# Low-weight products of the first layer on 49 rows each, in two halves of the array

## The chip, the cores and the metric

The kernel runs on one core of a Trainium2 chip. The metric is the device time of one execution, in microseconds (us); the kernel before takes 1061.57 us, the median of 3 runs (1059.65 to 1062.9). TensorE (PE) multiplies: it loads a stationary operand (the weights; the profile lists these loads as an engine of its own, PEld) and streams a moving operand past it. ScalarE (ACT) and VectorE (DVE) read its results from PSUM, in 8 banks, and write to SBUF.

## The reference

Two batches of 12480 tokens with 128 channels go through an attention with 49 agents, and its output goes through a layer with 2048 hidden features:

```python
a2k = sm(agents, k)          # softmax(scale * agents @ k.T), 49 x 12480
agent_v = a2k @ v            # 49 x 128
q2a = sm(q, agents)          # 12480 x 49
x = q2a @ agent_v
h = x @ w_in                 # 128 -> 2048
g = np.maximum(h, 0.0) + alpha * np.minimum(h, 0.0)
out = g @ w_out              # 2048 -> 128
```

## The kernel before

A first stage reads k and v, and forms `agent_v` of each batch. Since `h = q2a @ (agent_v @ w_in)`, the product M of `agent_v` and `w_in` (49 x 2048) is made once for each batch, so that the first layer has a contraction over 49 agents alone. To keep precision with float16 operands, M is split into a high and a low part, `M_a` and `M_b`, and so are the probabilities P. SBUF partitions 0 to 48 of `PT` hold the high part of P turned (agents by tokens), partitions 64 to 112 its low part (`LO` = 64, `A` = 49, `R` = 113). `M_a` holds the high part of M on both groups of partitions, `M_b` the low part on partitions 0 to 48, and zeros on the others, from a memset at the start. One product of 113 rows with `M_a` thus adds high x high and high x low, and one with `M_b` low x high.

The second stage, which takes most of the time, works through 52 chunks of 480 tokens. The features are 16 tiles of 128, in 8 pairs. For a pair PE issues, in the order in which the code is written: a wait for `lo_ready`, `first_layer` (L434: for the even and then the odd tile a product with `M_a` and one with `M_b`, each 480 columns long, into the banks 2g and 2g + 1), and `second_layer` of the pair two earlier (L442: six products of 128 rows by 480 columns: `w_hi`, `w_lo` with `r_hi`, and `w_hi` with `r_lo`, two of each). The increment of `h_ready` sits on the last product of `first_layer`. ACT then makes `r_hi` of both banks in one instruction (L614), and DVE `r_lo` (L825), whose increment of `lo_ready` lets PE write these banks again, two pairs later.

Once in a chunk, PE also issues the scores of the next chunk (L420, float32), the `linear` pair (L453), and four transposes of the split probabilities (L430, `stack`), which ACT copies from PSUM into `PT` (`query_out`, L604). That copy raises `q_ready`, for which PE waits ahead of the first layer of the next chunk and ahead of the scores. Every engine runs its instructions in the order written; loops (Fori) hold a body of two chunks.

A few products of the preparation have few rows and fall between those of the first chunk: L393 (`turn_values`, 49 rows), L399 (`values_max_row`, 49 rows, one column of weights), L404 (`values_max_everywhere`, one row) and L387 (`denominators`, 120 rows, 49 columns of weights).

Of the kernel before, what the change touches and what calls it, by code (L numbers as in the profile page):

```python
# [27 lines left out]
F16 = mybir.dt.float16  # L28
ALU = mybir.AluOpType
ACT = mybir.ActivationFunctionType  # L30
AX = mybir.AxisListType

B, N, C, A, F = 2, 12480, 128, 49, 2048
# [3 lines left out]
CHUNK = 4 * T  # L37
# [7 lines left out]
LO = 64  # L45
R = LO + A
# [6 lines left out]
def build(nc, kT, vP, qT, agT, w_in, w_inT, w_out, alpha_row, alpha_col, out):  # L53
    ctx = ExitStack()
    with ctx:
        def sb(name, shape, dt=F32):
            return ctx.enter_context(nc.sbuf_tensor(name, shape, dt))

        def sem(name):
            return ctx.enter_context(nc.semaphore(name))  # L60
# [44 lines left out]
        M_a = sb("M_a", [128, B, F], F16)  # L105
        M_b = sb("M_b", [128, B, F], F16)
# [13 lines left out]
        q_p = sb("q_p", [T, 4, A])  # L120
        stack = sb("stack", [T, 4, R], F16)
        PT = sb("PT", [128, 2, CHUNK], F16)
        r_hi = sb("r_hi", [128, RING, 2, CHUNK], F16)
        r_lo = sb("r_lo", [128, RING, 2, CHUNK], F16)
        y_lin = sb("y_lin", [C, 2, CHUNK])
# [5 lines left out]
        ps = ctx.enter_context(nc.psum_tensor("ps", [128, 8, 512], F32))  # L131
        OUT, LIN, SMALL = 4, 6, 7
# [25 lines left out]
        m_raw, m_high, m_low, l_raw, l_high, l_low = (  # L158
            sem(x) for x in ("m_raw", "m_high", "m_low", "l_raw", "l_high", "l_low"))

        q_scored, q_maxed, q_shifted, q_exped, q_summed, q_dened, q_reced, q_normed, q_hi, q_lo, q_turned, q_ready = (
            sem(x) for x in ("q_scored", "q_maxed", "q_shifted", "q_exped", "q_summed", "q_dened", "q_reced",
                             "q_normed", "q_hi", "q_lo", "q_turned", "q_ready"))
# [152 lines left out]
        def _(pe):  # L316
# [117 lines left out]
            def first_layer(g_even, p, half, b):  # L434
                for u in range(2):
                    f = 128 * (2 * p + u)
                    for w, last in ((M_a, False), (M_b, True)):
                        mm = pe.matmul(ps[:, 2 * g_even + u, 0:CHUNK], w[0:R, b, f:f + 128], PT[0:R, half, :],  # L438
                                       start=not last, stop=last)
                mm.then_inc(h_ready, 1)  # L440

            def second_layer(p, half):  # L442
# [8 lines left out]
            def linear(half, b):  # L451
                for w, last in ((L_a, False), (L_b, True)):
                    mm = pe.matmul(ps[:, LIN, 0:CHUNK], w[0:R, b, :], PT[0:R, half, :], start=not last, stop=last)  # L453
                mm.then_inc(lin_ready, 1)
# [28 lines left out]
            pe.wait_ge(m_low, 1)  # L483
            pe.wait_ge(l_low, 1)
            first_layer(0, 0, 0, 0)
            turn_values(1)
            first_layer(1, 1, 0, 0)

            pe.wait_ge(w_ready, 1)
# [60 lines left out]
        def _(act):  # L550
# [52 lines left out]

            def query_out(n, half):  # L604
                act.wait_ge(q_turned, n + 1)
                act.activation(PT[0:R, half, :], ps[0:R, SMALL, :].bitcast(F16)[:, 0:CHUNK], ACT.Copy).then_inc(q_ready, 1)

            def relu_hi(g, s, first):
                act.wait_ge(h_ready, g + 1)
# [50 lines left out]
        def _(dve):  # L660
# [93 lines left out]
            def values_max_top(b):  # L754
                dve.wait_ge(b_vrow, b + 1)
                then(dve.tensor_reduce(v_top[:, :], ps[0:1, AV_SMALL[b], 128:128 + A], AX.X, ALU.max))
                dve.tensor_scalar(v_top[:, :], v_top[:, :], TINY, None, ALU.max).then_inc(b_vtop, 1)
# [16 lines left out]
            def mixed_low(b, at, view, count):  # L774
                dve.wait_ge(m_high, count)
                n = view.shape[1]
                dve.tensor_tensor(M_b[0:A, b, at:at + n], view, M_a[0:A, b, at:at + n], ALU.subtract).then_inc(m_low, 1)

            def linear_low(b, bank):
                dve.wait_ge(l_high, b + 1)  # L780
                dve.tensor_tensor(L_b[0:A, b, :], ps[0:A, bank, 0:C], L_a[0:A, b, :], ALU.subtract).then_inc(l_low, 1)
# [5 lines left out]

            def mixed_low_first():
                linear_low(0, LIN)
                mixed_low(0, 0, ps[0:A, 0:4, :].rearrange("p f n -> p (f n)"), 1)  # L790

            def over_agents(x):
                return x.rearrange("p (t o) -> p t o", o=1).to_broadcast([T, 4, A])
# [3 lines left out]
            def query_shift(n):  # L797

                dve.wait_ge(q_scored, n + 1)
                dve.tensor_reduce(q_top[:, :], scores, AX.X, ALU.max).then_inc(q_maxed, 1)  # L800
                dve.wait_ge(q_maxed, n + 1)
                dve.tensor_tensor(q_e[:, :, :], scores, over_agents(q_top[:, :]), ALU.subtract).then_inc(q_shifted, 1)

            def query_sum(n):
                dve.wait_ge(q_exped, n + 1)
                dve.tensor_reduce(q_sum[:, :], q_e[:, :, :], AX.X, ALU.add).then_inc(q_summed, 1)
                dve.wait_ge(q_summed, n + 1)
                dve.tensor_scalar(q_den[:, :], q_sum[:, :], EPS, 1.0 / P_SCALE, ALU.add, ALU.mult).then_inc(q_dened, 1)
                dve.wait_ge(q_dened, n + 1)
                dve.reciprocal(q_rec[:, :], q_den[:, :]).then_inc(q_reced, 1)  # L810

            def query_norm(n):

                dve.wait_ge(q_reced, n + 1)
                dve.tensor_tensor(q_p[:, :, :], q_e[:, :, :], over_agents(q_rec[:, :]), ALU.mult).then_inc(q_normed, 1)

            def query_lo(n):
                dve.wait_ge(q_hi, n + 1)
                dve.tensor_tensor(stack[:, :, LO:R], q_p[:, :, :], stack[:, :, 0:A], ALU.subtract).then_inc(q_lo, 1)

            def relu_lo(g, s):

                dve.wait_ge(hi_ready, g + 1)
                e = s % 2
                dve.scalar_tensor_tensor(out=r_lo[:, s % RING, :, :], in0=ps[:, 2 * e:2 * e + 2, 0:CHUNK], scalar=0.0,  # L825
                                         in1=r_hi[:, s % RING, :, :], op0=ALU.max, op1=ALU.subtract).then_inc(lo_ready, 1)

            def finish(n, half, uses, unscale):

                dve.wait_ge(pair_done, PAIRS * n + PAIRS)  # L830
                dve.wait_ge(lin_saved, n + 1)
                if not (isinstance(uses, int) and uses == 0):

                    dve.wait_ge(stored[half], 16 * uses)
                dve.scalar_tensor_tensor(out=y[:, half, :], in0=ps[:, OUT + half, 0:CHUNK], scalar=unscale,
                                         in1=y_lin[:, half, :], op0=ALU.mult, op1=ALU.add).then_inc(y_ready, 1)
# [42 lines left out]
            def body(i, b, first, last):  # L879
                for half in range(2):  # L880
                    n = 2 * i + half
                    ahead = not (last and half == 1)
                    for p in range(PAIRS):
                        s = PAIRS * half + p
                        if p == 0 and ahead:
                            query_shift(n + 1)
                        if p == 1 and ahead:
                            query_sum(n + 1)
                            query_norm(n + 1)
                        if p == 2 and ahead:  # L890
                            query_lo(n + 1)
                        if ahead or p < PAIRS - 2:
                            relu_lo(2 * PAIRS * i + (s + 2), s + 2)
                        if isinstance(n, int) and n == 0:
                            if p == 1:
                                values_max_top(1)
                            if p == 2:
                                values_scaled(1)

                        if isinstance(n, int) and n == 0 and p == 4:  # L900
                            mixed_low(1, 3 * 512, ps[0:A, OUT + 1, :], 2)
                        if isinstance(n, int) and n < 3 and p == 5:
                            mixed_low(1, n * 512, ps[0:A, LIN, :], 3 + n)
                            if n == 0:
                                linear_low(1, SMALL)
                        if p == 3 and not (first and half == 0):

                            if half == 0:
                                finish(n - 1, 1, i - 1, prev_unscale[:, :])
                            else:  # L910
                                finish(n - 1, 0, i, out_unscale[:, b, :])
                        if p == 6 and half == 0 and not first:

                            dve.wait_ge(y_ready, n)
                            dve.tensor_copy(prev_unscale[:, :], out_unscale[:, b, :])
# [28 lines left out]
```

## Time and profile before

| | |
|---|---|
| median of 3 runs | 1061.57 us (1059.65 to 1062.9) |
| span of the profiled execution | 1057.5 us |
| PE busy, products | 1034.4 us (98%), 5800 instructions |
| PEld busy, weight loads | 579.0 us (55%) |
| DVE busy | 701.7 us (66%) |
| ACT busy | 518.5 us (49%) |
| one chunk of 480 tokens (602.77 to 620.39 us) | 17.62 us |

The profiled execution lists its span alone, 1057.5 us, from the first instruction of the program to the last; the median of the runs is 4.1 us above it, for what lies around the span. The shapes in a row read: `49*128` are the rows and columns of weights on the array, `49x113` the moving operand. The profile models the ends of products, and they overlap their successors; the distance from one start to the next tells what a product costs. Rows of the timeline merge equal neighbours (x2).

### The profile page before, as it was taken

The page shows a single profiled execution, that of the slowest core. Times are in us where ns is not written, and L with a number is a line of the kernel's source. Part 1 is how long each engine was busy: PE and PEld are TensorE (multiplying, and loading weights), DVE is VectorE, ACT ScalarE, POOL GpSimd, SP SyncE. Part 2 cuts the span into 40 slices and gives each one's busy share as a digit, 9 for nine tenths or more (in the row PEclk, how much of TensorE's full clock was granted, in tenths as well). Part 3 has the DMA queues.
Part 4 walks back from the last instruction along what each step waited for, and adds up shares of the span by engine and source line. Part 5 has one row for each costly group of instructions (what it writes and reads, how often), then busy time and mean ns, then how long its engine had stood idle before and what let it go on. Part 6 is the DMA issues. An engine that isn't in the chain of part 4 may idle for free.

```text
span 1057.5 us, 16185 instructions
## 1 busy us (share of the span) xinstructions
PE 1034.4 (98%) x5800; PEld 579.0 (55%) x5800; DVE 701.7 (66%) x991; ACT 518.5 (49%) x686; POOL 34.8 (3%) x27
## 2 busy tenths in 40 slices
PE   8978999999999999999999999999999999999998
PEld 8867855555555555555555555555555555555554
DVE  3686766666666666666666666666666666666665
ACT  2212355555555555555555555555555555555554
POOL 5070000000000000000000000000000000000000
PEclk9988999999999999999999999999999999999999
DMA  8877600101010101010101010101010101010100
GB/s 295 298 203 192 172 1 20 38 20 37 19 37 19 37 19 37 19 37 19 37 19 38 19 38 19 37 19 37 19 37 19 37 19 37 19 37 19 37 19 29
DMA packets 23116, 55.68 MB, mean 53 GB/s; under 512 B 2822, under 2 KB 16134, under 8 KB 22582
## 3 DMA queue, kind: packets, MB, share of 16 engines
q1 hardware_dynamic: 22806, 55.32, 17.0%
q8 instruction: 15, 0.25, 0.1%
q10 hardware_dynamic: 288, 0.06, 0.0%
q14 instruction: 7, 0.06, 0.0%
HBM read 42.59 MB, written 12.78 MB: 52 GB/s over the span
## 4 chain that ended last, share of the span: by engine, by line
PE 94%; DMA 3%; DVE 2%; ACT 0%; issue 0%; SPq 0%; DVEq 0%; ACTq 0%
PE ps L446 48%; PE ps L438 32%; PE ps L420 4%; PE ps L330 3%; PE ps L354 3%; PE ps L453 2%; DMA v_s<-vP 2%; PE ps L430 1%; DMA k_s<-kT 1%; PE ps L408 1%; DVE k_diag L689 1%; DMA agents<-agT 0%; DVE w_diag L729 0%; DVE S L699 0%; DVE r_lo L825 0%
## 5 line engine op out<-in xcount | busy, mean ns | idle before, releaser
L825 DVE SCALAR_TENSOR_TENSOR r_lo<-ps,r_hi 128x960 f16<-128x960 f32 x416 | 481.6, 1158 | 296.5 <-ACT r_hi L614 293.7
L614 ACT ACTIVATE r_hi<-ps 128x960 f16<-128x960 f32 x416 | 403.9, 971 | 431.5 <-PE ps L438 431.5
L438 PE MATMUL ps<-PT,M_a 113*128 113x480 f16 x832 | 304.3, 366 | 0.2 <-DVE r_lo L825 0.2
L438 PE MATMUL ps<-PT,M_b 113*128 113x480 f16 x832 | 303.0, 364 | 0.0
L446 PE MATMUL ps<-r_hi,w_hi 128*128 128x480 f16 x832 | 237.0, 365 | 0.0
L446 PE MATMUL ps<-r_lo,w_hi 128*128 128x480 f16 x832 | 236.5, 366 | 0.0
L446 PE MATMUL ps<-r_hi,w_lo 128*128 128x480 f16 x832 | 235.8, 365 | 0.0
L446 PEld LDWEIGHTS ps<-r_hi,w_hi 128*128 128x128 f16 x832 | 81.5, 98 | 87.5 <-DVE r_lo L825 0.3
L446 PEld LDWEIGHTS ps<-r_lo,w_hi 128*128 128x128 f16 x832 | 81.1, 97 | 87.4
L446 PEld LDWEIGHTS ps<-r_hi,w_lo 128*128 128x128 f16 x832 | 79.7, 96 | 89.0
L438 PEld LDWEIGHTS ps<-PT,M_a 113*128 113x128 f16 x832 | 83.5, 100 | 78.0 <-issue 0.5
L438 PEld LDWEIGHTS ps<-PT,M_b 113*128 113x128 f16 x832 | 81.1, 97 | 76.9 <-issue 0.7
L354 PE MATMUL ps<-v_s,e_s 120*49 120x128 f32 x416 | 52.6, 287 | 5.5 <-DMA v_s<-vP 3.3
L330 PE MATMUL ps<-agents,k_s 128*120 128x128 f32 x416 | 49.8, 284 | 7.1 <-DMA agents<-agT 4.6
L420 PEld LDWEIGHTS ps<-agents,q_s 128*120 128x120 f32 x416 | 51.7, 184 | 6.5 <-issue 0.2
L354 PEld LDWEIGHTS ps<-v_s,e_s 120*49 120x49 f32 x416 | 48.2, 131 | 9.0 <-DMA v_s<-vP 4.4
L330 PEld LDWEIGHTS ps<-agents,k_s 128*120 128x120 f32 x416 | 49.0, 193 | 7.5 <-DMA agents<-agT 4.6
L420 PE MATMUL ps<-agents,q_s 128*120 128x49 f32 x416 | 49.0, 261 | 0.0
L680 DVE TENSOR_REDUCE k_top<-S 120x49 f32<-120x392 f32 (+1 forms) x26 | 21.6, 833 | 30.3 <-ACT S L559 30.3
L572 ACT ACTIVATE e_s<-S 120x392 f32<-120x392 f32 (+1 forms) x26 | 13.6, 529 | 55.1 <-DVE S L699 51.1
L654 ACT ACTIVATE y_lin<-ps,lin_unscale 128x480 f32<-128x480 f32 x52 | 34.0, 654 | 0.0
L559 ACT ACTIVATE S<-ps 120x392 f32<-120x392 f32 (+1 forms) x26 | 12.9, 495 | 37.7 <-PE ps L330 37.7
(105 smaller groups left out, 452.5 us busy)
## 6 DMA issues: line engine op xcount, KB each, us to landing
k_s<-kT SPq DMA_DIRECT2D x26, 480.0 KB, 4.5
v_s<-vP SPq DMA_DIRECT2D x26, 480.0 KB, 5.6
q_s<-qT SPq DMA_DIRECT2D x52, 240.0 KB, 2.6
out<-y SPq DMA_DIRECT2D x52, 240.0 KB, 2.0
w_relu<-w_out SPq DMA_DIRECT2D x1, 1024.0 KB, 8.6
w_in_s<-w_in SPq DMA_DIRECT2D x1, 1024.0 KB, 7.5
w_inT_s<-w_inT SPq DMA_DIRECT2D x1, 1024.0 KB, 9.2
sigma<-alpha_row SPq DMA_DIRECT2D x1, 1024.0 KB, 8.3
```

What stands on the lines that cost most here:

```text
L330: mm = pe.matmul(ps[0:T, bank, t % 4 * 128:(t % 4 + 1) * 128], k_s[:, slot, t * T:(t + 1) * T], agents[:, :], start=True, stop=True)
L354: mm = pe.matmul(ps[0:A, AV[b], 0:C], e_s[:, slot, t * A:(t + 1) * A], v_s[:, slot, t * C:(t + 1) * C], start=(slot == RING and t == 0), s ...
L420: mm = pe.matmul(ps[0:T, SMALL, t * A:(t + 1) * A], q_s[:, half, t * T:(t + 1) * T], agents[:, b * A:(b + 1) * A], start=True, stop=True)
L438: mm = pe.matmul(ps[:, 2 * g_even + u, 0:CHUNK], w[0:R, b, f:f + 128], PT[0:R, half, :], start=not last, stop=last)
L446: mm = pe.matmul(ps[:, OUT + half, 0:CHUNK], w[:, 2 * p + u, :], r[:, s, u, :], start=(p == 0 and u == 0 and w is w_hi and r is r_hi), sto ...
L453: mm = pe.matmul(ps[:, LIN, 0:CHUNK], w[0:R, b, :], PT[0:R, half, :], start=not last, stop=last)
L559: act.activation(S[:, b, m, :].rearrange("p (t a) -> p t a", a=A), raw, ACT.Copy, scale=SCALE).then_inc(k_saved, 1)
L572: act.activation(e_s[:, slot, :], S[:, b, m, :], ACT.Exp).then_inc(k_exped, 1)
L614: act.activation(r_hi[:, s % RING, :, :], ps[:, 2 * e:2 * e + 2, 0:CHUNK], ACT.Relu).then_inc(hi_ready, 1)
L654: act.activation(y_lin[:, half, :], ps[:, LIN, 0:CHUNK], ACT.Copy, scale=lin_unscale[:, b, :]).then_inc(lin_saved, 1)
L680: dve.tensor_reduce(k_top[:, b, m, :], by_agent(S[:, b, m, :]), AX.X, ALU.max).then_inc(k_maxed, 1)
L825: dve.scalar_tensor_tensor(out=r_lo[:, s % RING, :, :], in0=ps[:, 2 * e:2 * e + 2, 0:CHUNK], scalar=0.0, in1=r_hi[:, s % RING, :, :], op0= ...
```

## The change

Three things change. In `first_layer` the two products with `M_a` come first, then the one with `M_b` of the even tile, on partitions 0 to 48, and then the one with `M_b` of the odd tile, on partitions 64 to 112. The odd one takes its moving operand from a new tile `PU`, whose partitions 64 to 112 hold a copy of the high part of P; ACT makes it in `query_out` by a second copy, which now carries the increment of `q_ready`. And the low part of M is made on all 113 partitions, by the same DVE instructions.

```diff
         PT = sb("PT", [128, 2, CHUNK], F16)
+        PU = sb("PU", [128, 2, CHUNK], F16)
...
             def first_layer(g_even, p, half, b):
                 for u in range(2):
                     f = 128 * (2 * p + u)
-                    for w, last in ((M_a, False), (M_b, True)):
-                        mm = pe.matmul(ps[:, 2 * g_even + u, 0:CHUNK], w[0:R, b, f:f + 128], PT[0:R, half, :],
-                                       start=not last, stop=last)
+                    pe.matmul(ps[:, 2 * g_even + u, 0:CHUNK], M_a[0:R, b, f:f + 128], PT[0:R, half, :],
+                              start=True, stop=False)
+                f = 256 * p
+                pe.matmul(ps[:, 2 * g_even, 0:CHUNK], M_b[0:A, b, f:f + 128], PT[0:A, half, :],
+                          start=False, stop=True)
+                mm = pe.matmul(ps[:, 2 * g_even + 1, 0:CHUNK], M_b[LO:R, b, f + 128:f + 256], PU[LO:R, half, :],
+                               start=False, stop=True)
                 mm.then_inc(h_ready, 1)
...
             def query_out(n, half):
                 act.wait_ge(q_turned, n + 1)
-                act.activation(PT[0:R, half, :], ps[0:R, SMALL, :].bitcast(F16)[:, 0:CHUNK], ACT.Copy).then_inc(q_ready, 1)
+                act.activation(PT[0:R, half, :], ps[0:R, SMALL, :].bitcast(F16)[:, 0:CHUNK], ACT.Copy)
+                act.activation(PU[LO:R, half, :], ps[0:A, SMALL, :].bitcast(F16)[:, 0:CHUNK], ACT.Copy).then_inc(q_ready, 1)
...
             def mixed_low(b, at, view, count):
...
-                dve.tensor_tensor(M_b[0:A, b, at:at + n], view, M_a[0:A, b, at:at + n], ALU.subtract).then_inc(m_low, 1)
+                dve.tensor_tensor(M_b[0:R, b, at:at + n], view, M_a[0:R, b, at:at + n], ALU.subtract).then_inc(m_low, 1)
```

The calls of `mixed_low` pass views of 113 partitions instead of 49.

On PE, in the second stage, one pair of tiles of the kernel before reads so (the first layer of a pair at L438, the second layer at L446):

```order
L438 MATMUL ps<-PT,M_a 128x480
L438 MATMUL ps<-PT,M_b 128x480
L438 MATMUL ps<-PT,M_a 128x480
L438 MATMUL ps<-PT,M_b 128x480
L446 MATMUL ps<-r_hi,w_hi 128x480 x2
L446 MATMUL ps<-r_hi,w_lo 128x480 x2
L446 MATMUL ps<-r_lo,w_hi 128x480 x2
```

The same place of the changed kernel, where L441 is the product of the even tile with `M_b`, L443 that of the odd tile, and L451 the second layer:

```order
L438 MATMUL ps<-PT,M_a 128x480 x2
L441 MATMUL ps<-PT,M_b 128x480
L443 MATMUL ps<-PU,M_b 128x480
L451 MATMUL ps<-r_hi,w_hi 128x480 x2
L451 MATMUL ps<-r_hi,w_lo 128x480 x2
L451 MATMUL ps<-r_lo,w_hi 128x480 x2
```

There are ten products in both; the product with `M_b` of the even tile has moved behind the one with `M_a` of the odd tile. (The shape here is that of the output, 128 features by 480 tokens; the rows of the array that a product uses are not in it.)

On ACT, around the copy of the turned probabilities, before (L614 makes `r_hi`, L654 `y_lin`, L606 `PT`):

```order
L614 ACTIVATE r_hi<-ps 128x960
L654 ACTIVATE y_lin<-ps,lin_unscale 128x480
L606 ACTIVATE PT<-ps 113x480
L609 REGISTER_ALU
L614 ACTIVATE r_hi<-ps 128x960
```

And changed, where the same instructions are at L620, L660 and L611:

```order
L620 ACTIVATE r_hi<-ps 128x960
L660 ACTIVATE y_lin<-ps,lin_unscale 128x480
L611 ACTIVATE PT<-ps 113x480
L612 ACTIVATE PU<-ps 49x480
L615 REGISTER_ALU
L620 ACTIVATE r_hi<-ps 128x960
```

One activation is added, between `PT` and the next `r_hi`.

## Rows read from the trace of the kernel before

**Rows 1.** The page, parts 1 and 2: engines' busy time; the granted clock
```profile
PE 1034.4 (98%) x5800; PEld 579.0 (55%) x5800; DVE 701.7 (66%) x991; ACT 518.5 (49%) x686; POOL 34.8 (3%) x27
...
PEclk9988999999999999999999999999999999999999
```

**Rows 2.** The page, part 4: the chain that ended last
```profile
PE 94%; DMA 3%; DVE 2%; ACT 0%; issue 0%; SPq 0%; DVEq 0%; ACTq 0%
PE ps L446 48%; PE ps L438 32%; PE ps L420 4%; PE ps L330 3%; PE ps L354 3%; PE ps L453 2%; DMA v_s<-vP 2%; PE ps L430 1%; DMA k_s<-kT 1%; PE ps L408 1%; DVE k_diag L689 1%; DMA agents<-agT 0%; DVE w_diag L729 0%; DVE S L699 0%; DVE r_lo L825 0%
```

**Rows 3.** The page, part 5: busy us, mean ns, idle before
```profile
L825 DVE SCALAR_TENSOR_TENSOR r_lo<-ps,r_hi 128x960 f16<-128x960 f32 x416 | 481.6, 1158 | 296.5 <-ACT r_hi L614 293.7
L614 ACT ACTIVATE r_hi<-ps 128x960 f16<-128x960 f32 x416 | 403.9, 971 | 431.5 <-PE ps L438 431.5
L438 PE MATMUL ps<-PT,M_a 113*128 113x480 f16 x832 | 304.3, 366 | 0.2 <-DVE r_lo L825 0.2
L438 PE MATMUL ps<-PT,M_b 113*128 113x480 f16 x832 | 303.0, 364 | 0.0
```

**Rows 4.** Timeline of PE, one pair: start us, length us, instruction
```profile
610.08 0.37 PE L438 MATMUL ps<-PT,M_a 113*128 113x480 f16 x1
610.29 0.36 PE L438 MATMUL ps<-PT,M_b 113*128 113x480 f16 x1
610.49 0.36 PE L438 MATMUL ps<-PT,M_a 113*128 113x480 f16 x1
610.69 0.36 PE L438 MATMUL ps<-PT,M_b 113*128 113x480 f16 x1
610.89 0.57 PE L446 MATMUL ps<-r_hi,w_hi 128*128 128x480 f16 x2
...
612.11 0.37 PE L438 MATMUL ps<-PT,M_a 113*128 113x480 f16 x1
```

**Rows 5.** Timeline of the weight loads around L399
```profile
139.30 0.08 PEld L399 LDWEIGHTS ps<-ident,v_col 49*1 49x1 f32 x2 [0.40 <-issue]
139.47 0.10 PEld L438 LDWEIGHTS ps<-PT,M_a 113*128 113x128 f16 x1
139.49 0.10 PEld L438 LDWEIGHTS ps<-PT,M_b 113*128 113x128 f16 x1
```

**Rows 6.** Timeline of the products around L399 (its second one)
```profile
139.01 0.36 PE L453 MATMUL ps<-PT,L_b 113*128 113x480 f16 x1
...
139.34 0.20 PE L399 MATMUL ps<-ident,v_col 49*1 49x49 f32 x1
139.48 0.38 PE L438 MATMUL ps<-PT,M_a 113*128 113x480 f16 x1
```

**Rows 7.** Timeline around L404: product ahead, its loads, the load behind
```profile
143.34 0.37 PE L446 MATMUL ps<-r_lo,w_hi 128*128 128x480 f16 x1
...
143.64 0.29 PEld L404 LDWEIGHTS ps<-v_top,ones 1*128 1x128 f32 x2 [0.40 <-issue]
...
143.74 0.18 PEld L404 LDWEIGHTS ps<-v_top,ones 1*128 1x128 f32 x1
143.94 0.10 PEld L438 LDWEIGHTS ps<-PT,M_a 113*128 113x128 f16 x1
```

**Rows 8.** Timeline around L420: product ahead, its loads, the load behind
```profile
174.32 0.57 PE L446 MATMUL ps<-r_lo,w_hi 128*128 128x480 f16 x2
...
174.53 1.02 PEld L420 LDWEIGHTS ps<-agents,q_s 128*120 128x120 f32 x8
175.40 0.16 PEld L438 LDWEIGHTS ps<-PT,M_a 113*128 113x128 f16 x1
```

**Rows 9.** Timeline of ACT and DVE at the copy into PT
```profile
608.31 0.57 ACT L606 ACTIVATE PT<-ps 113x480 f16<-113x480 f16 x1
609.07 0.97 ACT L614 ACTIVATE r_hi<-ps 128x960 f16<-128x960 f32 x1 [0.18 <-PE ps L438]
...
610.07 1.16 DVE L825 SCALAR_TENSOR_TENSOR r_lo<-ps,r_hi 128x960 f16<-128x960 f32 x1 [0.38 <-ACT r_hi L614]
```

**Rows 10.** Timeline of PE ahead of the first chunk
```profile
133.26 0.25 PE L387 MATMUL ps<-ones,k_col 120*49 120x1 f32 x2 [0.66 <-ACT PT L606]
```

More of the change, by code:

```diff
@@ L789, in mixed_low_first @@
                 linear_low(0, LIN)
-                mixed_low(0, 0, ps[0:A, 0:4, :].rearrange("p f n -> p (f n)"), 1)
+                mixed_low(0, 0, ps[0:R, 0:4, :].rearrange("p f n -> p (f n)"), 1)
             def over_agents(x):
@@ L900, in body @@
                         if isinstance(n, int) and n == 0 and p == 4:
-                            mixed_low(1, 3 * 512, ps[0:A, OUT + 1, :], 2)
+                            mixed_low(1, 3 * 512, ps[0:R, OUT + 1, :], 2)
                         if isinstance(n, int) and n < 3 and p == 5:
-                            mixed_low(1, n * 512, ps[0:A, LIN, :], 3 + n)
+                            mixed_low(1, n * 512, ps[0:R, LIN, :], 3 + n)
                             if n == 0:
```

## The prediction

> **What bounds the kernel now.** I read the page from the top. Products keep PE busy for 98% of the span, at the full clock once the second stage runs (the digits are 9, 90% or more; a window over 160 to 1050 us reads 1.00, which is the 2.4 GHz level) [rows 1]. The chain that ended last is 94% PE, with the second layer (L446) at 48% and the first (L438) at 32%; ACT has 0% and DVE 2%, of which `r_lo` has 0 [rows 2]. The groups say the same from the other side: DVE sat idle for 296.5 us ahead of its `r_lo` and ACT 431.5 us ahead of `r_hi`, waiting for what comes from PE, and PE waited for 0.2 us in all ahead of `M_a` products and 0.0 ahead of `M_b` [rows 3]. So every nanosecond by which a pair of tiles gets longer or shorter on PE goes to the end. In the timeline a pair repeats after 2.03 us (610.08 to 612.11) with ten products, so a product of 480 columns costs 0.203 us from start to start, whatever its rows: the busy length of 0.36 is no cost, as the next one starts inside it [rows 4].
>
> **What two products of 113 rows cost, and what could replace them.** Both `M_b` products of a pair take 2 x 0.203 = 0.406 us. If the two new ones stream at the same time on separate rows, they take one 0.203, and 0.203 x 416 pairs (52 chunks x 8) = 84 us would be gone. That is the gross gain, and it rests on two things: that both stream together, and that getting into and out of the split array costs nothing.
>
> **The second is what the trace can answer.** It has a few products of few rows among the wide ones. Ahead of L399 (49 rows, one column) the last wide product starts at 139.01, and the load for L399 only at 139.30: 0.29 us later, although weights are otherwise loaded under the product before. Behind it, the load of `M_a` starts at 139.47; the second L399 product started at 139.34 and streams for 0.04 (the distance of its two products, 139.30 to 139.34), so 0.13 - 0.04 = 0.09 us pass after its stream [rows 5, 6]. L404 (one row, 128 columns) tells the same: from 143.34 to its load at 143.64 are 0.30 us, against 0.203 for a stream; its second load starts at 143.74, 0.10 after the first, and the load of `M_a` comes at 143.94, 0.10 after that load could be over (143.84) [rows 7]. I need a control, since these are float32 products between float16 ones. L420 is that: float32 too, with 128 rows and 120 columns. Its load starts at 174.53, under the last of the two products of which the first began at 174.32 (0.203 later, so at once with it), and behind it the load of `M_a` comes without a hole (eight loads over 1.02 us, from 174.53 to 175.55, and the next one already at 175.40) [rows 8]. So the type is not the cause; the shape on the array is. The array runs empty for 0.09 us (0.29 - 0.203) before another shape is loaded, on the way in and on the way out.
>
> The Trainium skill, "TensorEngine Tiling (Array Packing)", section Key Properties, says that changing the tiling mode, and not just the tile, drains TensorE; by that rule, the trace agrees, with 0.09 us a drain. The same page, section Theoretical Speedup, promises up to 2x for a contraction of 64 or less; that is the rival "faster" below, and the two rules pull against each other here.
>
> **The sum for a pair.** Every first layer now has a wide part (`M_a`, 113 rows) and a split part (49 rows), followed by a wide one: two changes of shape in every pair, where before there was none.
> - Two drains: 2 x 0.09 = +0.18.
> - Loads that are no longer hidden. Behind a drain the load of `M_a` starts at 139.47, the next load at 139.49 and its product at 139.48 [rows 5, 6]: 0.01 to 0.02 us, I take 0.015. It happens for the even `M_b`, for `w_hi` behind the exit, and once more as the offset by which the odd one follows the even one: 3 x 0.015 = +0.045.
> - Streams: one of 0.203 in place of two: -0.203.
> Together +0.02 us a pair (0.18 + 0.045 - 0.203 = 0.022). Times 416: +9.2 us.
>
> Bounds. A drain lies between 0.09 and 0.10 in these rows: 0 to +0.02 a pair. The load of a 49-row float16 operand isn't in the trace. From below it can't cost less than nothing, -0.03 a pair for the two; from above the nearest rows are the float32 loads of 128 columns, 0.10 apart [rows 7], so +0.17 for the two exposed ones. I take the float16 row, as it has the same type and the same 128 columns. Whether both streams overlap isn't in the trace either: from 0 to a whole 0.203 more. I take the overlap, since the two use disjoint rows of the array and disjoint banks. The skill, "TensorE: Matmul & The Clock Gate", section Part 3, puts the offset of such streams at about 4 ns; by that estimate the pair would cost 0.011 us less and the kernel 4.6 us less than in my sum. No row here shows it.
>
> **The rest of the change.** The reordering of `M_a` and `M_b` within the first layer costs nothing: four products into two banks, ACT reads both banks together. The increment of `h_ready` comes a little earlier after the start of the pair (about 0.32 behind the odd `M_a` in place of 0.203, but that odd `M_a` stands one product earlier), so ACT and DVE lose nothing.
> The extra copy on ACT: `PT` takes 0.57 (608.31 to 608.88), and I take the same for `PU`, which has as many columns. It would end by 609.45 in place of a `r_hi` that started at 609.07, which comes 0.38 late at most. `r_lo` of that pair would then end at 610.07 + 1.16 + 0.38 = 611.61, and PE wants these banks at 612.11 [rows 4, 9]: 0.50 us of cover are left, so nothing. Without the cover it would be 0.38 x 52 = 20 us. `q_ready` is awaited two pairs behind the transposes (some 4 us), in which 0.57 is hidden too. Only ahead of the first chunk does it stand on the path: PE idles there for 0.66 until ACT has written `PT` [rows 10], so +0.5 once.
> `mixed_low` on 113 partitions has as many elements in each partition as before: nothing. L393, between the first two first layers, now meets the split shape on one side: -0.2 at most, once.
> All: 9.2 + 0.5 - 0.2 = 9.5 us. The profiled span of 1057.5 would become 1067.0. The median lies 4.1 us above the span, so I expect 1061.57 + 9.5 = 1071 us.
>
> **Rivals.**
> 1. The two streams don't overlap, or the 49-row load is slow. Serially there are still two streams of 0.203; the offset of the odd load is hidden then: 0.18 + 0.03 = +0.21 a pair, 87 us, 1149 us. With the slow load of 0.10 in place of 0.015, twice, but with overlap, it is 0.022 + 0.17 = +0.19, 79 us, 1141. For it: no row shows two products at once. Against: disjoint rows, disjoint banks. 18%, of which 4% for the load.
> 2. Faster: the switch doesn't drain between float16 products of 128 columns, or only on one side. With no drain the loads are hidden too, and a pair loses 0.203 less the offset of 0.015: -0.19, or -78 us, 983 us. One drain left: 0.022 - 0.09 - 0.015 = -0.08, or -35 us, 1027 us. It decides as soon as fewer than about 0.16 us of the 0.18 of drains are there. For it: each drain I read has a float32 product on one side. Against: the float32 product L420, of the wide shape, has none. 7%.
> 3. No change: drains and offsets at the low end (0.085 and 0.004 with hidden second load), so that a pair comes within 0.008 us of before. 8%.
> 4. ACT becomes late and PE waits once a chunk: it would add up to 20 us to my forecast. The cover of 0.50 speaks against it, and it is inside the 67% below with a weight of 3%.
>
> **How the numbers follow.** The overlap with drains has 67%: a pair from +0.01 to +0.04, 4 to 17 us, that is 1066 to 1078, and 1071 the likeliest. 0.3% (3.2 us) is about what a measurement of this kernel can tell from no change. Slower by more than that: 67 + 18 = 85%. Same: 8%. Faster: 7%. To hold 8 in 10 the range must take in the serial case, and so reaches from 1064 to 1151; what is left out is the faster rival and part of "no change". The likeliest case's own range is 1066 to 1078.
>
> **What would show it.** In the profile after, the `M_b` rows read 49*128; the two `M_b` products start within 0.02 us of each other (rival 1: 0.2 apart); the load for the even one starts 0.29 behind the odd `M_a`, and the load for `w_hi` 0.29 behind the odd `M_b`; a pair repeats after 2.05 us (rival 1: 2.24; rival 2: 1.84 or 1.95). PE's idle time ahead of `M_a`, released by DVE `r_lo`, stays under 1 us in all. I am wrong if the load for the even `M_b` starts under the odd `M_a`, or if the two products stand one behind the other.

## The result, and the profile after

The changed kernel takes 1064.52 us (median of 17 runs), the kernel before 1060.14 us in runs beside it (17). The ratio is 1.0041, 95% interval 1.0024 to 1.0059: slower by 4.4 us, where 9.5 were forecast. The direction and the mechanism were right, the size was not: less than half of it came.

Runs of one kernel spread by 6 to 11 us, and most of that goes with TensorE's granted clock, whose mean is listed for each run: over the 17 runs of the changed kernel and 55 of the kernel before (those beside the experiments) a straight line gives 0.8 us less for each 0.001 more of it. Taken at the same clock, the changed kernel lies 4.0 us (3.2 to 4.8) above the kernel before. In the profiled execution of the kernel before, the lower level of the clock shows only ahead of the second stage (a mean of 0.77 from 60 to 90 us, where PE is busy for 22 of the 30 us); from 160 us on every profile here reads 1.00, the 2.4 GHz level. Each run's time lies 1.8 us above its own span (1061.49 and 1059.7 in the profile after); the 4.1 us given earlier for what lies around the span thus hold some 2.3 us by which that one execution was faster than the median. The forecast of 9.5 us does not rest on them.

The page after, its parts 1 and 2 (busy time of the engines; the granted clock):

```profile
PE 1038.0 (98%) x5800; PEld 507.2 (48%) x5800; DVE 701.6 (66%) x991; ACT 551.2 (52%) x738; POOL 34.8 (3%) x27
...
PEclk9988999999999999999999999999999999999999
```

Against [rows 1], PE is as busy as before with the same 5800 products, ACT has 52 instructions more (the copies to `PU`), and the clock is the same. The chain (part 4) and the groups of part 5 that answer to [rows 2, 3]:

```profile
PE 95%; DMA 3%; DVE 1%; SPq 0%; issue 0%; ACT 0%; DVEq 0%; ACTq 0%
...
L831 DVE SCALAR_TENSOR_TENSOR r_lo<-ps,r_hi 128x960 f16<-128x960 f32 x416 | 481.6, 1158 | 298.6 <-ACT r_hi L620 295.5
L620 ACT ACTIVATE r_hi<-ps 128x960 f16<-128x960 f32 x416 | 404.0, 971 | 401.8 <-PE ps L443 400.5
...
L443 PE MATMUL ps<-PU,M_b 49*128 49x480 f16 x416 | 155.1, 373 | 0.0
L441 PE MATMUL ps<-PT,M_b 49*128 49x480 f16 x416 | 155.1, 373 | 0.0
...
L441 PEld LDWEIGHTS ps<-PT,M_b 49*128 49x128 f16 x416 | 38.6, 93 | 165.4 <-issue 165.4
...
L443 PEld LDWEIGHTS ps<-PU,M_b 49*128 49x128 f16 x416 | 38.6, 93 | 0.0
```

PE is still the bound, and DVE and ACT wait for it as before. New is the idle time of 165.4 us ahead of the 416 loads of L441: 0.40 us each, "issue", with no releaser. It is idle time of the load engine and not of the array, which still streams the odd `M_a` product through most of it. The loads of L443 have none. The loads of one pair (start us, length us):

```profile
611.12 0.09 PEld L441 LDWEIGHTS ps<-PT,M_b 49*128 49x128 f16 x1 [0.40 <-issue]
611.13 0.09 PEld L443 LDWEIGHTS ps<-PU,M_b 49*128 49x128 f16 x1
611.43 0.11 PEld L451 LDWEIGHTS ps<-r_hi,w_hi 128*128 128x128 f16 x2 [0.21 <-issue]
```

The load for the even `M_b` starts 0.29 behind the odd `M_a` product (610.83, see below), as forecast, and the load for `w_hi` 0.30 behind the `M_b` products (611.13), where 0.29 was forecast. Less a stream of 0.20, the array runs empty for 0.09 on the way in and 0.10 on the way out. The same pair in the timeline of the products (start us, length us), which answers to [rows 4]:

```profile
610.63 0.57 PE L438 MATMUL ps<-PT,M_a 113*128 113x480 f16 x2
611.13 0.37 PE L441 MATMUL ps<-PT,M_b 49*128 49x480 f16 x1
611.13 0.37 PE L443 MATMUL ps<-PU,M_b 49*128 49x480 f16 x1
611.44 0.58 PE L451 MATMUL ps<-r_hi,w_hi 128*128 128x480 f16 x2
611.85 0.57 PE L451 MATMUL ps<-r_hi,w_lo 128*128 128x480 f16 x2
612.26 0.57 PE L451 MATMUL ps<-r_lo,w_hi 128*128 128x480 f16 x2
612.66 0.57 PE L438 MATMUL ps<-PT,M_a 113*128 113x480 f16 x2
```

Both `M_b` products start at 611.13. The odd `M_a` product starts at 610.63 + 0.20, so 0.30 pass until 611.13, and 0.31 from there to 611.44: two steps of some 0.3 us stand where three of 0.203 were. From 610.63 to 612.66 is 2.03 or 2.04 us; hundredths don't resolve the loss. A chunk does: it is the distance from one group of scores to the next. There are 52 such groups, and the fourth and the last are 48 chunks apart. Before:

```profile
174.73 0.52 PE L420 MATMUL ps<-agents,q_s 128*120 128x49 f32 x4
...
1021.50 0.52 PE L420 MATMUL ps<-agents,q_s 128*120 128x49 f32 x4
```

and after:

```profile
173.63 0.52 PE L421 MATMUL ps<-agents,q_s 128*120 128x49 f32 x4
...
1023.61 0.52 PE L421 MATMUL ps<-agents,q_s 128*120 128x49 f32 x4
```

That is 846.77 / 48 = 17.641 us and 849.98 / 48 = 17.708 us: +0.067 a chunk, +0.0083 a pair, 3.5 us in 52 chunks. All chunk lengths below are made so, from the trace of each kernel. They agree between kernels to 0.001 us where nothing on PE changed, whereas the span also holds the first stage, which ends at other times in each execution (the first `M_a` product at 133.4 before, at 132.3 after).

The rest is the copy ahead of the first chunk:

```profile
132.12 0.25 PE L388 MATMUL ps<-ones,k_col 120*49 120x1 f32 x2 [1.23 <-ACT PU L612]
```

PE idles 1.23 us there, for `PU`, and 0.66 before [rows 10]: +0.57. With the 3.5 that makes 4.1 us, and 4.4 were measured. The interval of the measurement, 2.5 to 6.3 us, is much wider than that agreement.

### The profile page after: what moved, and what is told of

Read it like the earlier page. It is cut to its first block, busy times and chain, and to the rows that moved or that the text cites. A ratio compares the mean times of both kernels' runs of the same rounds, so it can differ in the third digit from the quotient of the medians.

```text
span 1059.7 us, 16237 instructions
## 1 busy us (share of the span) xinstructions
PE 1038.0 (98%) x5800; PEld 507.2 (48%) x5800; DVE 701.6 (66%) x991; ACT 551.2 (52%) x738; POOL 34.8 (3%) x27
## 4 chain that ended last, share of the span: by engine, by line
PE 95%; DMA 3%; DVE 1%; SPq 0%; issue 0%; ACT 0%; DVEq 0%; ACTq 0%
PE ps L451 52%; PE ps L438 16%; PE ps L441 12%; PE ps L421 4%; PE ps L355 3%; PE ps L331 3%; PE ps L458 2%; DMA v_s<-vP 2%; PE ps L431 1%; DMA k_s<-kT 1%; PE ps L409 1%; DVE k_diag L695 1%; DMA agents<-agT 0%; DVE S L705 0%; DVE w_diag L735 0%
## 5 line engine op out<-in xcount | busy, mean ns | idle before, releaser
L831 DVE SCALAR_TENSOR_TENSOR r_lo<-ps,r_hi 128x960 f16<-128x960 f32 x416 | 481.6, 1158 | 298.6 <-ACT r_hi L620 295.5
L620 ACT ACTIVATE r_hi<-ps 128x960 f16<-128x960 f32 x416 | 404.0, 971 | 401.8 <-PE ps L443 400.5
L451 PE MATMUL ps<-r_hi,w_hi 128*128 128x480 f16 x832 | 240.7, 371 | 0.0
L438 PE MATMUL ps<-PT,M_a 113*128 113x480 f16 x832 | 236.9, 365 | 0.0
L451 PE MATMUL ps<-r_hi,w_lo 128*128 128x480 f16 x832 | 236.5, 366 | 0.0
L451 PE MATMUL ps<-r_lo,w_hi 128*128 128x480 f16 x832 | 236.5, 366 | 0.0
L443 PE MATMUL ps<-PU,M_b 49*128 49x480 f16 x416 | 155.1, 373 | 0.0
L441 PE MATMUL ps<-PT,M_b 49*128 49x480 f16 x416 | 155.1, 373 | 0.0
L451 PEld LDWEIGHTS ps<-r_hi,w_lo 128*128 128x128 f16 x832 | 81.4, 98 | 87.3
L451 PEld LDWEIGHTS ps<-r_lo,w_hi 128*128 128x128 f16 x832 | 81.4, 98 | 87.1
L441 PEld LDWEIGHTS ps<-PT,M_b 49*128 49x128 f16 x416 | 38.6, 93 | 165.4 <-issue 165.4
L438 PEld LDWEIGHTS ps<-PT,M_a 113*128 113x128 f16 x832 | 79.2, 102 | 66.0 <-issue 1.2
L451 PEld LDWEIGHTS ps<-r_hi,w_hi 128*128 128x128 f16 x832 | 47.2, 97 | 88.6 <-issue 88.2
L443 PEld LDWEIGHTS ps<-PU,M_b 49*128 49x128 f16 x416 | 38.6, 93 | 0.0
```

The source lines that it names most:

```text
L438: pe.matmul(ps[:, 2 * g_even + u, 0:CHUNK], M_a[0:R, b, f:f + 128], PT[0:R, half, :], start=True, stop=False)
L441: pe.matmul(ps[:, 2 * g_even, 0:CHUNK], M_b[0:A, b, f:f + 128], PT[0:A, half, :], start=False, stop=True)
L443: mm = pe.matmul(ps[:, 2 * g_even + 1, 0:CHUNK], M_b[LO:R, b, f + 128:f + 256], PU[LO:R, half, :], start=False, stop=True)
L451: mm = pe.matmul(ps[:, OUT + half, 0:CHUNK], w[:, 2 * p + u, :], r[:, s, u, :], start=(p == 0 and u == 0 and w is w_hi and r is r_hi), sto ...
L620: act.activation(r_hi[:, s % RING, :, :], ps[:, 2 * e:2 * e + 2, 0:CHUNK], ACT.Relu).then_inc(hi_ready, 1)
```

## The experiments

| kernel | chunk, us | time, us | ratio to before (95%) |
|---|---|---|---|
| before | 17.641 | 1060 | |
| changed | 17.708 | 1064.5 | 1.0041 (1.0024 to 1.0059) |
| e1_order | 17.641 | 1061.5 | 1.0011 (0.999 to 1.0031) |
| e3_wide_with_copy | 17.641 | 1063.0 | 1.0019 (1.0 to 1.0037) |
| e4_even_only | 17.681 | 1064.0 | 1.0032 (1.0007 to 1.0056) |
| e2_same_half | 19.298 | 1145.8 (one run) | |
| e5_apart | 20.978 | 1241.9 (one run) | |
| v1_one_shared | 17.444 | 1051.5 | 0.9928 (0.9908 to 0.9949) |
| v2_two_shared | 17.523 | 1060.1 | 1.0001 (0.9989 to 1.0012) |
| v5_one_between | 17.313 | 1047.0 | 0.9871 (0.9837 to 0.9906) |
| v6_two_between | 17.383 | 1052.9 | 0.9925 (0.9894 to 0.9956) |
| v4_all_shared | 18.691 | 1118.5 | 1.0567 (1.0542 to 1.0592) |

**The order alone.**

```diff
-                for u in range(2):
-                    for w, last in ((M_a, False), (M_b, True)):
+                for w, last in ((M_a, False), (M_b, True)):
+                    for u in range(2):
```

> Only the order of the four first-layer products changes (both with M_a, then both with M_b), all still 113 rows. Theory (the time of a pair is starts of 0.203 us plus changes of shape): no change, a pair stays at 2.03 us, within 0.3% of before. Rival (part of the loss is the reordering itself, for instance two loads or two products of one operand in a row): +0.007 us a pair, about +3 us, as in the changed kernel.

The chunk is 17.641, as before to the last digit. The reordering costs nothing; the rival, which would have made +0.06 a chunk, falls.

**The copy alone.** The changed kernel with the four products of before in `first_layer`.

```diff
-                    pe.matmul(ps[:, 2 * g_even + u, 0:CHUNK], M_a[0:R, b, f:f + 128], PT[0:R, half, :],
...
+                    for w, last in ((M_a, False), (M_b, True)):
+                        mm = pe.matmul(ps[:, 2 * g_even + u, 0:CHUNK], w[0:R, b, f:f + 128], PT[0:R, half, :],
+                                       start=not last, stop=last)
```

> The products of the kernel before (113 rows, old order), with the second copy by ACT and the low part of M on 113 partitions. Theory (the copy is hidden but for the one ahead of the first chunk): +0.5 us on before, a pair 2.03 us. Rival (the copy makes PE wait once a chunk): up to 0.38 x 52 = 20 us; or it accounts for the whole +4 us of the change.

The chunk is 17.641 again: the copy is hidden in every chunk. The ratio of 1.0019 can't tell 0.5 us from the 3 us above before, and its interval touches no change; the chunk says that nothing of it is paid chunk by chunk. These runs had a lower clock on average (0.991 against 0.993), and in the profile the first chunks ran at it (0.77 from 135 to 150 us); taken at the same clock, they lie 0.9 us above before, with an interval from 0 to 1.9. How ACT looks at that place in the changed kernel:

```profile
608.79 0.57 ACT L611 ACTIVATE PT<-ps 113x480 f16<-113x480 f16 x1
609.37 0.56 ACT L612 ACTIVATE PU<-ps 49x480 f16<-49x480 f16 x1
609.96 0.97 ACT L620 ACTIVATE r_hi<-ps 128x960 f16<-128x960 f32 x1
...
610.96 1.16 DVE L831 SCALAR_TENSOR_TENSOR r_lo<-ps,r_hi 128x960 f16<-128x960 f32 x1 [0.84 <-ACT r_hi L620]
```

`r_hi` starts at 609.96, right behind `PU`, where it had a hole of 0.18 ahead of it before [rows 9]. `r_lo` ends at 612.12, and PE takes these banks at 612.66: 0.54 us of cover, where I had worked out 0.50.

**Do the two halves stream at once?** The odd product put on the rows of the even one:

```diff
-                mm = pe.matmul(ps[:, 2 * g_even + 1, 0:CHUNK], M_b[LO:R, b, f + 128:f + 256], PU[LO:R, half, :],
+                mm = pe.matmul(ps[:, 2 * g_even + 1, 0:CHUNK], M_b[0:A, b, f + 128:f + 256], PT[0:A, half, :],
```

> The changed kernel, but the odd tile's product with M_b also uses rows 0 to 48, like the even one. Theory (the two halves stream at once in the changed kernel): here they stream one behind the other, starts 0.21 us apart, a pair takes 2.23 to 2.24 us, the time is about 1064 + 0.20 x 416 = 1148 us. Rival (the starts 4 ns apart in the profile are only issue times, and the array does one after the other anyway, with the drains hidden): within 5 us of the changed kernel.

1145.8 us: the theory. Its timeline:

```profile
612.22 0.37 PE L441 MATMUL ps<-PT,M_b 49*128 49x480 f16 x1
612.43 0.36 PE L443 MATMUL ps<-PT,M_b 49*128 49x480 f16 x1
612.73 0.58 PE L451 MATMUL ps<-r_hi,w_hi 128*128 128x480 f16 x2
```

The products start 0.21 apart here, 0.00 in the changed kernel, and the chunk grows by (19.298 - 17.708) / 8 = 0.199 us a pair. The overlap is real, and worth one stream. It also gives the price of the change of shape by itself, since as many streams as before are left: (19.298 - 17.641) / 8 = 0.207 us a round trip.

**Does the second half cost anything?** The odd `M_b` product left out (the result lacks that low part). The odd `M_a` product then ends its bank, and the increment of `h_ready` sits on the even `M_b` product; all else is as in the changed kernel:

```diff
-                mm = pe.matmul(ps[:, 2 * g_even + 1, 0:CHUNK], M_b[LO:R, b, f + 128:f + 256], PU[LO:R, half, :],
-                               start=False, stop=True)
```

> The changed kernel without the odd tile's product with M_b: its low part of M is left out. Theory (the second half streams inside the first): the time falls by the offset alone, 0.0035 us x 416 = 1.5 us, a pair 2.03 us. Rival (the two streams slow each other): it falls by more, by up to 0.2 x 416 = 84 us.

The chunk loses 17.708 - 17.681 = 0.027 us, 0.0033 a pair. So that is the offset between two products in different halves of the array; the second product is otherwise free. The trace of the changed kernel, read in whole nanoseconds, says the same: the odd `M_b` product starts 3 or 4 ns behind the even one, in all of the 386 pairs read behind 200 us.

**Is the price paid for every change of shape?** Each `M_b` product directly behind its `M_a`, in its own half, four changes of shape a pair:

> The changed kernel, but each M_b product of 49 rows directly behind its M_a, so that the shape changes four times a pair, and nothing overlaps. Theory (each round trip costs 0.207): a pair 2.03 + 0.41 = 2.44 us, about 1060 + 172 = 1232 us. Rival (a drain is paid only once in some time, or is hidden by the loads of the next): less than 1200 us.

```diff
...
                 f = 256 * p
+                pe.matmul(ps[:, 2 * g_even, 0:CHUNK], M_a[0:R, b, f:f + 128], PT[0:R, half, :],
+                          start=True, stop=False)
                 pe.matmul(ps[:, 2 * g_even, 0:CHUNK], M_b[0:A, b, f:f + 128], PT[0:A, half, :],
                           start=False, stop=True)
+                pe.matmul(ps[:, 2 * g_even + 1, 0:CHUNK], M_a[0:R, b, f + 128:f + 256], PT[0:R, half, :],
+                          start=True, stop=False)
                 mm = pe.matmul(ps[:, 2 * g_even + 1, 0:CHUNK], M_b[LO:R, b, f + 128:f + 256], PU[LO:R, half, :],
                                start=False, stop=True)
```

The loop that made the two `M_a` products is gone; the arguments of the four calls are the same.

```profile
612.21 0.37 PE L437 MATMUL ps<-PT,M_a 113*128 113x480 f16 x1
612.51 0.37 PE L439 MATMUL ps<-PT,M_b 49*128 49x480 f16 x1
612.82 0.38 PE L441 MATMUL ps<-PT,M_a 113*128 113x480 f16 x1
613.13 0.37 PE L443 MATMUL ps<-PU,M_b 49*128 49x480 f16 x1
```

Every start comes 0.30 or 0.31 after the last, in place of 0.203. The chunk grows by 3.337, 0.417 a pair, 0.209 for each of two round trips. 1241.9 us against the expected 1232; 52 x 3.337 = 174 is the forecast 172, and of the other 9 us 5.4 lie ahead of the first chunk (the first `M_a` product at 138.8 us, 133.4 before) and 3.7 in the first three, where this one execution was granted a clock of 0.67 from 135 to 150 us (1.00 before). The rival falls.

**Sharing the switch.** If 0.207 is a fixed price and each pair of tiles gives back 0.203, two pairs in one split stretch win 0.2 us. In one place of a chunk, the other six pairs as before the change (but with the low part of M on all 113 rows):

```diff
+                        if p in (0,):
+                            for k in range(2):
+                                pe.wait_ge(lo_ready, g + 1 + k)
+                                first_high(k, p + 2 + k, half, b)
+                            for k in range(2):
+                                first_low(k, p + 2 + k, half, b)
```

with the `linear` pair moved ahead of it. `first_high` has the two `M_a` products, `first_low` the two split ones of the changed kernel.

> Split products in one place of a chunk only, where two pairs share one change of shape: scores and linear first, then the M_a products of both pairs, then the four M_b products of both (49 rows), then both second layers; the other six pairs have the wide products of before. Theory (a change to the split shape and back costs 0.207 us, whatever streams inside; each pair of tiles in it saves one stream of 0.203): a chunk goes from 17.64 to 17.64 - 2 x 0.203 + 0.207 = 17.44 us, 10 us less than before, about 1050 us. Rival (the drain grows with what is inside, or PE must wait for r_lo since two pairs now start together): a chunk stays at 17.6 or more.

```profile
613.99 0.97 PE L446 MATMUL ps<-PT,M_a 113*128 113x480 f16 x4
614.89 0.37 PE L451 MATMUL ps<-PT,M_b 49*128 49x480 f16 x1
614.89 0.37 PE L453 MATMUL ps<-PU,M_b 49*128 49x480 f16 x1
615.10 0.36 PE L451 MATMUL ps<-PT,M_b 49*128 49x480 f16 x1
615.11 0.36 PE L453 MATMUL ps<-PU,M_b 49*128 49x480 f16 x1
615.40 0.58 PE L461 MATMUL ps<-r_hi,w_hi 128*128 128x480 f16 x2
```

The chunk is 17.444, forecast 17.44, and the time 1051.5 us, forecast about 1050; the ratio is 0.9928. This version beats both kernels. In two places:

```diff
-                        if p in (0,):
+                        if p in (0, 4):
```

with `linear` moved to the second one, behind the transposes, and `y_lin` on ACT from p = 3 to p = 5.

> The same in two places of a chunk, the second behind the transposes and the linear pair, which is moved there to give ACT and DVE time. Theory: a chunk 17.64 - 4 x 0.203 + 2 x 0.207 = 17.24 us, 21 us less than before, about 1039 us. Rival (a wait of PE for r_lo takes the place of what is saved): the idle time ahead of the M_a products released by DVE r_lo rises above 5 us in all, and the time stays above the version with one place.

The chunk is 17.523 and not 17.24, and no time is won. Of the 0.118 us that a chunk is still shorter than before, 6 us in all, the first chunks give more than half back, since behind the later `linear` three products of the preparation wait for `y_lin`:

```profile
PE ps L409 <- ACT y_lin L671: 3.3, 3, 1.4
```

(The columns are us in total, times, and the longest.) The profile counts only 1.9 us of idle time of PE ahead of the `M_a` products for `r_lo`, so my mark of 5 us was not met, and yet the wait is there. In PE's rows it hides in the lengths:

```profile
607.05 1.24 PE L446 MATMUL ps<-PT,M_a 113*128 113x480 f16 x4
608.22 0.37 PE L451 MATMUL ps<-PT,M_b 49*128 49x480 f16 x1
...
606.49 1.16 DVE L849 SCALAR_TENSOR_TENSOR r_lo<-ps,r_hi 128x960 f16<-128x960 f32 x1 [0.87 <-ACT r_hi L637]
```

Four `M_a` products take 1.24 here and 0.97 in the version with one place. `r_lo` ends at 607.65, and the third product may not start earlier. From the second to the third product 0.46 us pass in place of 0.20, a wait of 0.25. A product is listed as busy for 0.37 but leaves room for the next after 0.20, so 0.17 of the wait is no idle time in the profile, and what is left, 0.09, is shorter than any idle time that its views list. The load engine does show the wait, because its loads are listed with 0.1 us and end well ahead of the next:

```profile
PEld ps L446 <- DVE r_lo L849: 45.1, 104, 1.3
```

In the version with one place the same wait is 0.9 us, in 2 loads. That line is the mark that should have been set. One product of the second layer between the two pairs of `M_a` should cover it, and `linear` stays in place in the first three chunks:

```diff
                                 first_high(k, p + 2 + k, half, b)
+                                if p == 4 and k == 0 and 1:
+                                    second_layer(p, half, 0, 1)
...
-                        second_layer(p, half)
+                        second_layer(p, half, 1 if p == 4 else 0)
```

> The version with two shared places, whose second place waited 0.2 us a chunk for the second r_lo (616.0 to 616.9 in the first place is nearly free of it). Here one product of the second layer is issued between the M_a products of the two pairs in the second place, which covers 0.20 of that wait; and the linear pair stays where it was in the first three chunks. Theory (the wait is for banks that come free a fixed time after, so work in front of it covers it): a chunk 17.52 - 0.20 = 17.32 us and some 3 us less in the first chunks, about 1044 us. Rival (everything behind is later by as much, the wait moves to the next first layer): a chunk stays at 17.5 us, about 1054 us.

```profile
602.79 0.36 PE L449 MATMUL ps<-PT,M_a 113*128 113x480 f16 x1
603.00 0.37 PE L465 MATMUL ps<-r_hi,w_hi 128*128 128x480 f16 x1
...
603.25 0.58 PE L449 MATMUL ps<-PT,M_a 113*128 113x480 f16 x2
603.76 0.37 PE L454 MATMUL ps<-PT,M_b 49*128 49x480 f16 x1
```

17.313 us a chunk, forecast 17.32, 1047.0 us in time, forecast about 1044, and a ratio of 0.9871: 1.3% faster than the kernel before, the best here. With two products between (`second_layer(p, half, 0, 2)`):

> The same with two products between. Theory: the rest of the wait (0.06) is covered too, but the M_b products of the first pair come 0.4 us later, and the next first layer, which had 0.37 us of slack behind r_lo, has none: a chunk 17.26 to 17.32 us, 1041 to 1044 us. Rival as for one product.

17.383 us, worse than with one, and worse than the range I gave. In its next first layer `M_a` comes 0.49 after two products that take 0.41:

```profile
626.56 0.57 PE L465 MATMUL ps<-r_lo,w_hi 128*128 128x480 f16 x2
627.05 0.38 PE L442 MATMUL ps<-PT,M_a 113*128 113x480 f16 x1
```

The slack of 0.37 was used up, and a wait of 0.09 us a chunk moved there, as feared; the chunk is 0.06 above the top of my range. Against the version with one product between, the chunk accounts for 3.6 of the 5.9 us. The runs of this version also had the lower clock (0.9885 on average against 0.9915); why is open, so the chunk and not the time ranks the two.

**All pairs shared.**

```diff
-                        if p in (0, 4):
+                        if p % 2 == 0:
```

(the group at p = 6 goes to the next chunk, and there is none in the last.)

> All eight pairs two by two, also where no other work of PE lies between. Theory by shape changes alone: 17.64 - 8 x 0.203 + 4 x 0.207 = 16.84 us a chunk, 1018 us. With the turnaround of the banks (from the first M_b start 0.41 us until r_hi, 1.00 until r_lo, 1.16, and 1.1 for the r_lo of the second pair: 3.67, and 0.5 until the next M_b): 4.19 us for two pairs at least, where the work is 3.85, so two places without other work wait 0.34 each: 17.5 us a chunk, 1054 us, and more where ACT and DVE have other work between.

1118.5 us, far over both. The waits of PE:

```profile
PE ps L446 <- DVE r_lo L852: 75.8, 103, 1.3
```

and the place where they are:

```profile
613.30 0.57 PE L446 MATMUL ps<-PT,M_a 113*128 113x480 f16 x2
615.13 0.58 PE L446 MATMUL ps<-PT,M_a 113*128 113x480 f16 x2 [1.26 <-DVE r_lo L852]
```

Two places of a chunk have no other work of PE between. One waits about 0.34 in start to start (0.54 in place of 0.20), the number I had worked out; the other waits 1.42 (from the second product at 613.51 to 615.13 is 1.62). DVE shows what makes the difference:

```profile
611.77 1.16 DVE L852 SCALAR_TENSOR_TENSOR r_lo<-ps,r_hi 128x960 f16<-128x960 f32 x1 [1.37 <-ACT r_hi L640]
612.85 0.34 DVE L833 TENSOR_REDUCE q_sum<-q_e 120x4 f32<-120x196 f32 x1
...
613.64 0.36 DVE L842 TENSOR_TENSOR q_p<-q_e,q_rec 120x196 f32<-120x196 f32 x1
613.92 1.15 DVE L852 SCALAR_TENSOR_TENSOR r_lo<-ps,r_hi 128x960 f16<-128x960 f32 x1
```

Between the `r_lo` of the two pairs stand four instructions of the next chunk's softmax (ACT had the second `r_hi` ready at 612.86), and they put the second one off by 1.07 us (612.85 to 613.92), which is the 1.08 by which the two waits differ. I had given the softmax no time in that stretch. No run has these four moved elsewhere.

## Why the prediction was off

- *PE alone sets the time*: right. DVE waits by the same sum as before (298.6 us ahead of `r_lo`), ACT by 30 us less, which is the time of its 52 copies to `PU`.
- *The array runs empty on a change of shape, 0.09 in and 0.09 out*: right, 0.09 and 0.10 measured. It was read from three odd products of the preparation with a control, and holds for float16 products of 480 columns. Rival 2 (faster, no drain between float16 products) is refuted by e5_apart and by the loads of L441, which start 0.29 behind the odd `M_a` product and never under it.
- *The 49-row load is as fast as the float16 load of 113 rows*: right; the round trip is 0.207, and 0.18 + 2 x 0.015 had been put in for it. The slow load of rival 1 would have shown as +0.17 a pair.
- *Both halves stream at once*: right, against the main part of rival 1, by e2_same_half. The rule of the Trainium skill, "TensorE: Matmul & The Clock Gate", Part 3, that such streams start about 4 ns apart agrees with this case: 0.0033 us a pair by e4_even_only.
- *"Once more as the offset by which the odd one follows the even one"*: this is the step that failed. I took 0.015 us, the price of an exposed load, for what two loads in different halves do not pay: it measured 0.0033. That is 0.0117 of the 0.0137 by which the pair was put too high. The rest is the round trip, 0.180 + 0.030 in the sum and 0.207 measured, or 0.208 in the changed kernel (0.0025), less 0.0005 for a stream of 0.2025 that I took as 0.203. Together the pair costs 0.0083 and not 0.022, the second stage 3.5 us and not 9.2. The term of 0.015 was a twelfth of each of the big terms, but these cancel (0.207 against 0.203), so that the remainder is made of just such small terms.
- *The copy is hidden but for the first*: right, 0.57 against 0.5, and no change of the chunk in e3_wide_with_copy. *L393 gains 0.2 at most*: it gained nothing that can be seen, its load waits for DVE (in the trace after, its product starts 0.44 behind the split ones).
- *Rival 3 (no change)*: it was nearest to what came. Its offset of 0.004 is what the runs show. Its drains of 0.085 are not (0.09 and 0.10), so that the pair, at 0.0083, comes out just above its 0.008 and just below the 0.01 at which my likeliest case began. I had given it 8%, though I had a figure for the offset at hand (the 4 ns of the Trainium skill) that I kept out of the sum; by my estimate with it, 4.6 us less, the forecast would have been 4.9 us.
- *The range, 1064 to 1151 us*: the 1064.52 lies at its very bottom, under the 1066 to 1078 of the likeliest case. It had been stretched upward for the serial case, which did not come; that it holds the time says little for the sum.

## What to carry to other kernels

A change of the array's shape cost 0.207 to 0.209 us for the way in and out in this kernel, with streams of 480 columns around it, and with one, two or four products of 49 rows in between (the version with one shared place fits that price to 0.01); packing two products of few rows into one stream gives back 0.199. So pack only where at least two such streams share one switch, and look then at who must free the banks early: here one shared place won 0.7%, two with one product put in front of the wait 1.3%, and all of them lost 5.7%.

When two large terms of a sum cancel, the forecast is no better than the sum of their roundings: read them to the nanosecond, over many repeats (a chunk of the loop, 48 times), and widen the range about "no change".

## What the runs showed of the hardware that was not expected

- The distance between two products of 49 rows in different halves of the array, loads included, is 0.0033 us. The second load runs beside the first (611.12 and 611.13, 0.09 us each), so it is not waited for although no stream hides it.
- The length of a product in the profile (0.36 to 0.38 us for 480 columns, of which 0.20 is its place in the stream) swallows waits of up to 0.17 us. The version with two shared places lost 0.28 us a chunk against its forecast with 1.9 us of PE's idle time listed in the whole run; the starts of the products tell, and so does the idle time of the load engine (45.1 us, released by `r_lo`).
- A chunk's length repeats to 0.001 us between kernels with the same work on PE (before, e1_order, e3_wide_with_copy), while the runs of one kernel spread by 6 to 11 us. An effect of 0.0033 us on an instruction could be read that way, though the run times could not have shown it.
